# Opening of a fused RWKV-attention and MLP kernel: GpSimd's r·k products wait for all decays, and scores and masks of the first two batches are grouped ahead of bonus sums and diagonals

## The reference, cut to what matters

```
for t in range(S):
    kt, vt, rt = k[:, :, t], v[:, :, t], r[:, :, t]
    cur = einsum('bhd,bhe->bhde', u[None] * kt, vt)
    y[:, :, t] = einsum('bhd,bhde->bhe', rt, state + cur)
    state = w[None, :, :, None] * state + einsum('bhd,bhe->bhde', kt, vt)
```

## Time and profile before

| | us |
|---|---|
| median of 3 runs (lowest, highest) | 873.17 (872.77, 875.27) |
| the profiled execution, its own time | 872.39 |
| span of the profiled execution | 870.6 |
| PE busy | 862.8 (99%) |
| ACT, DVE, POOL busy | 368.4, 348.1, 238.0 |

### The profile page before, as it was taken

One profiled execution on the slowest core, in us unless ns is written; L12 is line 12 of the kernel. 1 busy time (PEld: TensorE's weight loads), 2 busy tenths in 40 slices (PEclk: granted clock), 3 DMA queues, 4 the chain that ended last, 5 costly groups with the idle time before them and its releaser, 6 DMA issues.

```text
span 870.6 us, 13166 instructions
## 1 busy us (share of the span) xinstructions
PE 862.8 (99%) x5074; PEld 712.8 (82%) x5074; DVE 348.1 (40%) x521; ACT 368.4 (42%) x679; POOL 238.0 (27%) x213
## 2 busy tenths in 40 slices
PE   8999999999999999999999999999999999999998
PEld 7998888887888888777888888888888888888886
DVE  7756245324433452433243433333433333333333
ACT  4543232232223222322465754445644446544444
POOL 6969314222241332131175411002220003100000
PEclk9999999999999999999999999999999999999999
DMA  9554212312320422221223000000100000100001
GB/s 269 159 193 127 70 54 74 83 46 64 96 77 20 116 76 64 58 71 26 84 74 114 31 1 1 0 1 1 73 1 0 2 1 0 73 1 1 1 0 73
DMA packets 38128, 49.56 MB, mean 57 GB/s; under 512 B 5905, under 2 KB 30354, under 8 KB 38066
## 3 DMA queue, kind: packets, MB, share of 16 engines
q1 hardware_dynamic: 37536, 48.52, 19.2%
q10 hardware_dynamic: 530, 0.20, 0.1%
HBM read 36.11 MB, written 4.72 MB: 47 GB/s over the span
## 4 chain that ended last, share of the span: by engine, by line
PE 97%; DVE 1%; DMA 1%; issue 1%; SPq 0%; ACT 0%; POOL 0%; DVEq 0%; ACTq 0%; POOLq 0%
PE h L1322 23%; PE acc L1350 22%; PE h L1393 21%; PE acc L1494 11%; PE pair L1494 8%; PE a_bank L1494 4%; PE a_bank L1206 3%; PE pair L1239 2%; PE pair L1252 1%; PE a_bank L1264 1%; DMA arena<-in_rk 1%; DVE arena L982 0%; DVE arena L1014 0%; DVE arena L1030 0%; SPq L414 0%
## 5 line engine op out<-in xcount | busy, mean ns | idle before, releaser
L1322 PE MATMUL h<-xs,win_hi 128*128 128x512 f32 (+1 forms) x636 | 178.5, 378 | 0.5 <-DVE g_lo L1072 0.5
L1072 DVE TENSOR_TENSOR g_lo<-h,g_hi 128x512 fp32r<-128x512 f32 (+1 forms) x106 | 67.8, 640 | 235.1 <-ACT g_hi L756 235.1
L1322 PEld LDWEIGHTS h<-xs,win_hi 128*128 128x128 f32 x636 | 111.8, 188 | 23.1 <-issue 1.6
L1140 DVE TENSOR_TENSOR g_lo<-arena,g_hi 128x512 fp32r<-128x512 f32 x96 | 66.9, 697 | 133.4 <-ACT g_hi L882 133.4
L752 ACT ACTIVATE h<-h 128x512 f32<-128x512 f32 (+1 forms) x106 | 57.5, 542 | 137.4 <-PE h L1322 134.2
L756 ACT ACTIVATE g_hi<-h 128x512 fp32r<-128x512 f32 (+1 forms) x106 | 59.1, 557 | 125.8 <-PE acc L1350 125.2
L1133 DVE TENSOR_TENSOR arena<-h,arena 128x512 f32<-128x512 f32 x96 | 66.4, 692 | 102.6 <-ACT arena L895 85.8
L553 POOL TENSOR_TENSOR arena<-arena 112x1024 f32<-112x1024 f32 x20 | 47.8, 2388 | 194.0 <-DMA arena<-in_rk 188.2
L879 ACT ACTIVATE arena<-arena 128x512 f32<-128x512 f32 x96 | 60.7, 632 | 93.9 <-DVE arena L1133 93.9
L895 ACT ACTIVATE arena<-h 128x512 f32<-128x512 f32 x96 | 56.5, 589 | 80.7 <-PE h L1393 80.3
L1350 PE MATMUL acc<-g_hi,wout_hi 128*128 128x512 f32 (+1 forms) x318 | 85.0, 369 | 0.0
(11 more groups left out here) (163 smaller groups left out, 1375.8 us busy)
## 6 DMA issues: line engine op xcount, KB each, us to landing
mid<-in_wts SPq DMA_DIRECT2D x24, 384.0 KB, 5.7
arena<-in_rk SPq DMA_DIRECT2D x46, 192.0 KB, 3.4
xs<-xt SPq DMA_DIRECT2D x117, 48.0 KB, 2.0
arena<-in_k SPq DMA_DIRECT2D x22, 192.0 KB, 3.8
arena<-in_r SPq DMA_DIRECT2D x22, 192.0 KB, 4.1
arena<-in_v SPq DMA_DIRECT2D x22, 192.0 KB, 3.9
arena<-in_wts SPq DMA_DIRECT2D x8, 384.0 KB, 3.2
out<-mid SPq DMA_DIRECT2D x4, 768.0 KB, 3.3
```

The lines of the kernel that those rows point to most:

```text
L1072: dve.tensor_tensor(g_lo[:, g % 2, cols], h_cols(g), f32(g_hi[:, g % 2, cols]), ALU.subtract).then_inc(glo_done, 1)
L1140: dve.tensor_tensor(g_lo[:, g % 2], h_of(n), f32(g_hi[:, g % 2]), ALU.subtract).then_inc(glo_done, 1)
L1322: ins = pe.matmul(hb, w[:, f, kd, :], x_part(lo, par, kd)[:, c0:c1], start=i + kd == 0, stop=i == 2 and kd == KD - 1)
```

## The change

GpSimd's two products wait until all four decay halves are done (`r_first` 4), also the product of unit 0. On DVE both units' masks come ahead of both diagonals. On TensorE both scores come ahead of both bonus sums, and one `keep_warm` matmul into `acc` 0 stands behind each scores.

```diff
             def product(n):
 
-                pool.wait_ge(r_first, 2 * (n + 1))
+                pool.wait_ge(r_first, 2 * EARLY)
                 pool.tensor_tensor(rk_prod[n], first[n].rk[:, 0], first[n].rk[:, 1], ALU.mult).then_inc(prod_done, 1)
...
             for n in range(EARLY):
                 select(n)
+            for n in range(EARLY):
                 diagonal(n)
...
             scores(0)
+            keep_warm(acc[0], 1)
+            scores(1)
+            keep_warm(acc[0], 1)
             early_sums(0)
-            scores(1)
             early_sums(1)
             inside(0)
             inside(1)
```

## The result

The changed kernel takes 876.38 us (median of 21 runs; a single slow run of 2209.5 us is left out, with it the median is 876.45), the kernel before 872.70 us (22 runs) in the same rounds: ratio 1.0034, 95% interval 1.0026 to 1.0041. By that ratio it is slower by some 3 us; the medians lie 3.7 apart, because four of its runs are at 872.9 to 873.4 and the other seventeen at 876.0 to 877.6. The forecast was 873.0 with a range to 874.9.

The account below looks back on a forecast made before the run. TensorE's matmul issue (99% busy) was taken as the bound, with only the opening open to change. inside(1) ending at 17.14 instead of 17.28 gives 873.17 - 0.14 = 873.03 us, range 871.7 to 874.9.

Parts of the forecast that it names:

- The opening is all that the change can touch, and TensorE's rest shifts with it: Only 8.09 to 17.28 us, some 9 us, can change; everything behind shifts as much as the end of inside(1).
- The third decay half goes from 1.64 to 0.68, the first mask starts at 10.04: On DVE: 0.97 us saved on the decays, of which 0.22 is left because the first mask needs unit 0's scores.
- the bound was the one forecast: The first mask on DVE waits for TensorE's scores of unit 0, which end at 9.99, not for the decays.
- The step that failed: TensorE's opening: keep_warm issue 0.13 to 0.25 us, up to 0.4, scores(1) 0.98, bonus sums(0) 1.16; inside(0) at 13.91.
- Rival 3, the clock, 0.06: TensorE's clock falls in the new idle stretch before inside(0): +4.5 us, 877.5 in all; chance 0.06.
- The rest of the sum: From inside(0) at 13.91 to inside(1) ending at 17.14 instead of 17.28: 0.14 us gained, span 870.5.
- up to 0.1 late, hidden: DVE's low part of the second weight block, 0.88 us, ends up to 0.1 late, hidden behind `up(0)`.
- Bonus sums as the bound (rival 1): Slow third decay not GpSimd's doing, bonus sums(0) bind, inside(1) ends at 17.54: +0.26 us, 873.4; chance 0.12.

Follow-up runs that it names:

- second_warm_only: The changed kernel with only the keep_warm behind scores(1), the one behind scores(0) removed; median 875.50 us.
- pool_only: The kernel before with only GpSimd's wait of the change, so unit 0's product waits for all four decay halves; median 874.95 us.
- pe_order_only: The kernel before with only TensorE's new order, both scores ahead of both bonus sums, without keep_warm; median 875.18 us.
- no_warm: The changed kernel without its two keep_warm matmuls; median 873.74 us.
- dve_order_only: The kernel before with only DVE's new order, both masks ahead of both diagonals; median 875.77 us, 872.85 in a second set.

## Why the prediction was wrong

- *The opening is all that the change can touch, and TensorE's rest shifts with it*: right. Transposes +3.45 us, span +3.6.
- *The third decay half goes from 1.64 to 0.68, the first mask starts at 10.04*: right for the decays (both halves 1.29 together). The mask at 10.10 in the changed kernel agrees by luck: the transfer of unit 1 was 0.7 us late, and the decays ended only at 10.07. But in the trace of second_warm_only they end at 9.17, and DVE waits 0.93 us for scores(0), until 10.10: the bound was the one forecast.
- *The step that failed*: "0.13 to 0.25 of issue, up to 0.4 if it still runs at the slow rate of scores(0)" for the keep_warm, then 0.98 for scores(1) and 1.16 for sums(0). These are durations of the fast rate, and the 0.4 of the slow one was too small too. I had read in the earlier trace rows that the clock rises between 9.8 and 10.8, and carried that moment over into a kernel in which the stream there is another. In the changed kernel the two keep_warm hold TensorE 0.73 and 0.72 us, scores(1) 2.0, the sums 1.87 and 1.85 to the next start. Diagonal(0) starts at 15.51, not 12.5, and inside(0) waits, behind the sums of unit 1, until 17.10, not 13.91. That is 3.2 us; a slow first half of inside(0) is the other 0.3.
- *Rival 3, the clock, 0.06*: the right engine and about the right size (it said +4.5 us, the medians say +3.7), but the wrong event. I looked for a fall in the new idle stretch before inside(0); what happened is that the rise, near 10 in the trace I had, came at 17.8. The argument against it, that 0.92 us of pause brought no fall before, says nothing on a rise. The sentence of the Trainium skill that I cited (TensorE: Matmul & The Clock Gate, Part 1) has both halves of it: activity lifts the clock, and the moment varies from run to run. The traces agree with the second half: 9.9 and 12.4 in two executions of one kernel.
- *The rest of the sum*: where the clock was up in time it held. In the trace of second_warm_only inside(0) starts at 13.96 (forecast 13.91) and the transposes at 17.13 (17.14). Yet its span is 870.8, where 870.5 was forecast. There a second, small step failed: "up to 0.1 late, hidden". DVE's low part of the second weight block took 1.65 us, not 0.88, beside GpSimd's low parts (one begins at 16.89 and takes 1.00); the low part of unit 1 then ended at 18.78, and the nine matmuls of `up(0)` took 1.49 us in the chain instead of 1.25. The four early runs of the change itself (872.90 to 873.38) aren't below the 872.70 of the kernel before either. So even with the early rise no gain shows.
- *Bonus sums as the bound (rival 1)*: by place it is right, diagonal(0) does wait 1.46 us for them, but because TensorE is slow; the products were done at 12.65 (forecast 11.97, the late transfer is in it) and TensorE came to the sums at 13.38.

What stays open is what exactly TensorE has to do for the rise. That a keep_warm or a fill behind the scores makes it late more often is shown by counts; for a pause (pool_only, pe_order_only) and for the order the counts are too few. But no_warm's trace shows overlapping matmul records from 2 to 18.9 us, all slow, and the trace of dve_order_only has its rise at 14.6, with the same TensorE stream up to there as the kernel before. No rule that I could form from these traces fits all of them.

## What to carry to other kernels

While TensorE is still at its slow rate, price every piece of its opening at that rate (here 0.42 against 0.27 us a matmul, 0.73 us for one keep_warm between groups of 48-row matmuls), and ask whether the edit changes the stream before the rise, not only whether it makes a pause after. The moment of the rise isn't a property of a kernel that one trace can show: take two traces, and many runs. A keep_warm belongs into a wait that is there anyway, ahead of the first dependent work; between two pieces of real work it costs its own time and, in most runs here, the early rise.

## What the runs showed of the hardware that I had not expected

- The column of granted clock said 1.00 throughout the opening, also where the matmuls' durations (417 ns against 272) show the lower level. The level's own records begin only with the rise (10.06, 12.51 and 17.94 us in the two traces of the kernel before and in that of the change), and the durations agree with them.
- One keep_warm (two records) between 48-row matmuls takes 0.73 us at the slow rate, where four in a row take 2.0 us, 0.5 each.
- DVE's low part, with two SBUF operands, took 1.65 us in second_warm_only beside two GpSimd instructions (the rest of one to 16.93, then one of 1.00 us), where another of the same shape takes 0.54.
- Executions of one kernel fall into clusters some microseconds apart (the change: 872.9 to 873.4, then 876.0 to 877.6), and a set of six runs can lie wholly above the early one.
